# The general attention path's code moved ahead of the banded one's, and the first expert tiles of a two-layer mixture of experts listed half a slot sooner

## The reference

```python
def _attn_ref(q, k, v, n_global, n_local):
    scores = scale * q @ k.T                      # per batch and head
    keep = (pos_k < n_global) | ((rel >= 0) & (rel < n_local))
    scores = np.where(keep, scores - slope[h] * dist, -1e9)
    a = exp(scores - max); a = a / (sum(a) + 1e-09)
    return a @ v

def _moe_ref(x, w_gate, w1, w2):                  # x: 3072 rows of 512
    logits = x @ w_gate                           # 8 experts
    expert_idx = argmax(logits); gate_w = softmax(logits)[expert_idx]
    for e in range(8):
        xe = x[expert_idx == e]
        out[expert_idx == e] = gate_w * (relu(xe @ w1[e]) @ w2[e])
```

## Time and profile before

| | us |
|---|---|
| median of 3 executions | 1014.54 |
| the profiled execution | 1014.87 |
| its span, first to last instruction | 1013.2 |
| outside the span | 1.7 |
| attention, until PE's last attention matmul ends | 279.2 |
| handover, from there to the first down product | 11.0 |
| the rest: two mixtures and what lies between | 723 |

### The profile page before, as it was taken

The page is one execution under the profiler, slowest core; times in us unless marked ns, Lnnn a source line. Parts: engine busy times, 40 slices in busy tenths (PEclk is TensorE's granted clock), DMA queues, the critical chain, the costliest instruction groups (busy, mean ns, idle before and its releaser), DMA issues.

```text
span 1013.2 us, 18862 instructions
## 1 busy us (share of the span) xinstructions
PE 956.1 (94%) x5383; PEld 810.9 (80%) x5384; DVE 609.3 (60%) x1625; ACT 387.9 (38%) x715; POOL 194.7 (19%) x263
## 2 busy tenths in 40 slices
PE   5999999999989999999999999369999999999994
PEld 4999999999868888888888888257888888888883
DVE  5666666667688979879897978872322234222241
ACT  4555555654424433525333333232322233222230
POOL 2002830000122312122221210021221112111110
PEclk9999999999899999999999999779999999999998
DMA  9977974740223515333452515013311115111110
GB/s 166 180 154 186 279 150 98 151 144 17 64 101 140 199 50 207 124 124 126 145 185 77 182 40 199 21 31 115 125 41 45 48 44 197 41 41 41 41 42 9
DMA packets 138412, 110.73 MB, mean 109 GB/s; under 512 B 101839, under 2 KB 114175, under 8 KB 138240
## 3 DMA queue, kind: packets, MB, share of 16 engines
q1 hardware_dynamic: 125808, 74.46, 27.5%
q0 software_dynamic: 11072, 35.69, 10.4%
q10 hardware_dynamic: 1488, 0.04, 0.1%
HBM read 87.36 MB, written 23.33 MB: 109 GB/s over the span
## 4 chain that ended last, share of the span: by engine, by line
PE 90%; DVE 4%; issue 2%; DMA 2%; ACT 1%; DVEq 0%; SPq 0%; POOL 0%; POOLq 0%; ACTq 0%
PE PS L1469 29%; PE PS L1449 29%; PE PS L364 8%; PE PS L342 7%; PE PS L1457 4%; PE PS L352 4%; PE PS L1438 2%; PE PS L299 2%; PE PS L328 2%; PE PS L319 1%; DMA k_rows<-in_k_dram 1%; DMA xin<-attended,early_rows 1%; PE PS L1237 0%; PE PS L1482 0%; DMA xin<-mixed,gather_rows 0%
## 5 line engine op out<-in xcount | busy, mean ns | idle before, releaser
L1449 PE MATMUL PS<-W,xT_high 128*128 (+1 forms) x864 | 272.5, 396 | 3.6 <-DVE xT_low L1617 2.8
L1469 PE MATMUL PS<-W,hT_high 128*128 (+1 forms) x848 | 270.9, 400 | 0.8 <-DVE hT_low L1624 0.8
L1449 PEld LDWEIGHTS PS<-W,xT_high 128*128 128x128 f32 x864 | 159.0, 189 | 35.1 <-issue 3.9
L1469 PEld LDWEIGHTS PS<-W,hT_high 128*128 128x128 f32 x848 | 155.2, 188 | 34.8 <-DVE hT_low L1624 1.0
L1449 PE MATMUL PS<-W,xT_low 128*128 (+1 forms) x432 | 169.3, 392 | 0.0
L1469 PE MATMUL PS<-W,hT_low 128*128 (+1 forms) x424 | 167.6, 395 | 0.0
L1571 ACT ACTIVATE hT_high<-PS 128x512 fp32r<-128x512 f32 x110 | 59.8, 596 | 273.5 <-PE PS L1457 246.5
L1644 DVE CUSTOM_DVE_ANT_0 products<-y,gate_columns 128x512 f32<-128x512 f32 x224 | 141.0, 685 | 0.1
L589 ACT ACTIVATE pbuf<-biased_scores,nmax 128x256 f32<-128x256 f32 (+1 forms) x192 | 87.3, 488 | 105.5 <-DVE nmax L447 104.4
L1566 ACT ACTIVATE h<-PS 128x512 f32<-128x512 f32 x110 | 65.5, 597 | 161.3 <-PE PS L1449 157.6
L1617 DVE TENSOR_TENSOR xT_low<-PS,xT_high 128x512 fp32r<-128x512 f32 x56 | 38.6, 689 | 139.3 <-ACT xT_high L1560 139.0
(11 more groups left out here) (283 smaller groups left out, 1119.5 us busy)
## 6 DMA issues: line engine op xcount, KB each, us to landing
stage<-in_moe_w_dram SPq DMA_DIRECT2D x80, 512.0 KB, 5.5
mixed<-y POOLq DMA_DIRECT2D x30, 256.0 KB, 2.3
q_rows<-in_q_dram SPq DMA_DIRECT2D x32, 192.0 KB, 3.9
k_rows<-in_k_dram SPq DMA_DIRECT2D x32, 192.0 KB, 4.3
v_rows<-in_v_dram SPq DMA_DIRECT2D x32, 192.0 KB
attended<-x_rows SPq DMA_DIRECT2D x16, 384.0 KB, 3.3
v_before<-in_v_dram SPq DMA_DIRECT2D x32, 150.0 KB
stage<-in_moe_w_dram POOLq DMA_DIRECT2D x8, 512.0 KB, 9.3
```

What stands on the lines that cost most here:

```text
L1449: last = pe.matmul(t.PS[:, f, :], lhs[:, c, :], t.W[:, bass.ds(w + part, 512)], start=c == 0 and n == 0, stop=c == KD - 1 and n == 2)
L1469: last = pe.matmul(t.PS[:, 2, :], lhs[:, c, :], t.W[:, bass.ds(off + (c * D + part), D)], start=c == 0 and n == 0, stop=c == KF - 1 and n ...
```

## The change

- The general path's code stands ahead of the banded one on SP, PE, DVE and ACT. Each engine reads the flag once (`path`), ahead of both. What PE and ACT did ahead of the flag (the first transposes and their moves, the waits on constants) is now inside the banded branch; DVE's mask tables (L176 to L182 of the kernel before) become `distances`, called inside the branch. `last_logits` is the end of the banded DVE function.
- `preview_rows` and `preview` part 7 go from slot (3,7) to the end of slot (3,6).
- `turn_first(0)` goes from behind the weighing of head 6 in slot (8,0) to ahead of it, and `x_low_first` on DVE from behind the move of the probabilities to ahead of `finish`. ACT does `x_high_first` ahead of all four parts of `spread_gate2` rather than behind the first.
- The 8 steps of `up_first` stand as 0, 1 / 2 in slot (8,0) and 3, 4 / 5 in slot (8,1), and 6, 7 behind it; before it was none / 0, 1 and 2, 3 / 4, and 5, 6, 7.

```diff
+def path(eng, t, s):
+    eng.wait_ge(s.flag_ready, 1)
+    return eng.to_reg(eng.value_load(t.banded[0:1, 0:1], min_val=0, max_val=1))
...
-    def tensor(pe):
+    def tensor(pe, flag):
...
-        pe.wait_ge(s.ident_made, 2)
-        transpose_qk(0, 0, True, range(4))
-        pe.wait_ge(s.consts, CONSTS)
-        pe.wait_ge(s.qT_cleared, 2)
-        pe.wait_ge(s.small_loaded, 48)
-        pe.wait_ge(s.flag_ready, 1)
-        flag = pe.value_load(t.banded[0:1, 0:1], min_val=0, max_val=1)
-        with pe.If_eq(pe.to_reg(flag), 1):
+        with pe.If_eq(flag, 1):
+            pe.wait_ge(s.ident_made, 2)
+            transpose_qk(0, 0, True, range(4))
+            pe.wait_ge(s.consts, CONSTS)
+            pe.wait_ge(s.qT_cleared, 2)
+            pe.wait_ge(s.small_loaded, 48)
...
+                if not has_h and has_g:
+                    pe.wait_ge(s.xT_moved, 2 * NPR * B - 1)
+                    turn_first(t, s, pe, 0)
                 if has_f:
                     pe.wait_ge(s.pT_moved, 3 * H * b + 2 + 3 * f + 3)
-                    if last and h == 7:
-                        preview_rows(t, s, pe)
                     weigh_v(f % H, range(2, NQ)).then_inc(s.weighed, 1)
                 if not has_h and has_g:
-                    pe.wait_ge(s.xT_moved, 2 * NPR * B)
-                    turn_first(t, s, pe, 0)
                     rank_count(t, s, pe)
                 if not has_h and not has_g:
-                    up_first(t, s, pe, range(2, 4))
+                    up_first(t, s, pe, range(3, 5))
...
                     transpose_p(b, g, 1)
+                    if not has_h:
+                        up_first(t, s, pe, range(0, 2))
...
+                if last and h == 6:
+                    pe.wait_ge(s.logits_moved, NPR * b + 3)
+                    preview_rows(t, s, pe)
                 if has_g:
                     transpose_p(b, g, 2)
...
                 if not has_h:
-                    up_first(t, s, pe, range(0, 2) if has_g else range(4, 5))
+                    up_first(t, s, pe, range(2, 3) if has_g else range(5, 6))
...
-            up_first(t, s, pe, range(5, 2 * KD))
+            up_first(t, s, pe, range(6, 2 * KD))
...
-    def vector(dve):
-        flag = dve.value_load(t.banded[0:1, 0:1], min_val=0, max_val=1)
-        with dve.If_eq(dve.to_reg(flag), 1):
+    def vector(dve, flag):
+        with dve.If_eq(flag, 1):
+            distances(dve)
             dve.sem_inc(s.biased, 3)
...
-                if last and h == 7:
-                    dve.wait_ge(s.weighed, H * b + f + 1)
-                    preview(t, s, dve, 7)
+                if not has_h and has_g:
+                    x_low_first(t, s, dve)
                 if has_f:
                     finish(b, f)
...
                 if not has_h and has_g:
-                    x_low_first(t, s, dve)
                     rank(t, s, dve, 1)
...
+                if last and h == 6:
+                    preview(t, s, dve, 7)
...
             modality(t, s, dve)
+            now = t.logits[:, (B - 1) * NQ:B * NQ, :]
+            dve.wait_ge(s.logits_read, NPR * B)
...
                 if not has_h and has_g:
-                    spread_gate2(act, t, s, range(0, 1))
                     x_high_first(t, s, act)
-                    spread_gate2(act, t, s, range(1, 4))
+                    spread_gate2(act, t, s, range(0, 4))
...
         @block.vector
         def _(dve):
             first_dve(dve)
-            banded_dve(dve)
-            general_dve(dve)
-            last_logits(dve)
+            flag = path(dve, t, s)
+            general_dve(dve, flag)
+            banded_dve(dve, flag)
```

More of the change, by code:

```diff
@@ L98, in sync @@
         sp.sem_inc(s.rows_loaded, 1)
-        sp.wait_ge(s.flag_ready, 1)
     def gpsimd(pool):
@@ L175, in vector, with distances, link @@
         dve.wait_ge(s.tables, TABLES)
+        dve.wait_ge(s.consts, CONSTS)
+    def distances(dve):
+        n = [6]
+        ng, nl = t.parf[:, 0:1], t.parf[:, 1:2]
+        def link(ins):
+            n[0] += 1
+            ins.then_inc(s.setup_chain, 1)
+            dve.wait_ge(s.setup_chain, n[0])
         dist, lost = t.tmp[:, 0, :], t.tmp[:, 2, :]
@@ L247, in gpsimd, with sync @@
         pool.wait_ge(s.x2_cleared, 16 * (MAXT - NT))
-    def sync(sp):
-        flag = sp.value_load(t.banded[0:1, 0:1], min_val=0, max_val=1)
-        with sp.If_eq(sp.to_reg(flag), 1):
+    def sync(sp, flag):
+        with sp.If_eq(flag, 1):
             def load(b, p):
@@ L548, in vector, with scalar @@
             modality(t, s, dve)
-    def scalar(act):
+            now = t.logits[:, (B - 1) * NQ:B * NQ, :]
+            dve.wait_ge(s.logits_read, NPR * B)
+            dve.wait_ge(s.logits_moved, NPR * B)
+            dve.tensor_tensor(now, now, t.ps_lg[:, 0:NQ * E].rearrange("p (i e) -> p i e", e=E), ALU.add)\
+               .then_inc(s.logits_moved, 1)
+            dve.wait_ge(s.logits_moved, NPR * B + 1)
+    def scalar(act, flag):
         def move_qk(b, p, units):
@@ L566, in move_qk @@
                 last.then_inc(s.qk_moved, 1)
-        act.sem_inc(s.qk_moved, 2)
-        move_qk(0, 0, range(4))
-        act.wait_ge(s.consts, CONSTS)
-        act.wait_ge(s.flag_ready, 1)
-        flag = act.value_load(t.banded[0:1, 0:1], min_val=0, max_val=1)
-        with act.If_eq(act.to_reg(flag), 1):
+        with act.If_eq(flag, 1):
+            act.sem_inc(s.qk_moved, 2)
+            move_qk(0, 0, range(4))
+            act.wait_ge(s.consts, CONSTS)
             act.sem_inc(s.exped, 3)
@@ L600, in scalar, with sync @@
             run_slots(act, slot)
[L602 to L612 removed]
+    return gpsimd, sync, tensor, vector, scalar
 def general_attention(t, s, q, k, v, x1, w_gate2):
     qf, kf, vf = (a.rearrange("b h (i p) d -> (b h) p i d", p=P) for a in (q, k, v))
[L619 to L621 removed]
+    def sync(sp, flag):
+        with sp.If_eq(flag, 0):
             sp.sem_inc(s.rows_loaded, 1)
[L624 removed]
             with sp.Fori(0, B) as b:
@@ L642, in sync, with tensor @@
                 sp.dma_start(t.x[:, 0, :], x1[bass.ds(i * P, P), :]).then_inc(s.g_x, 16)
-    def tensor(pe):
-        flag = pe.value_load(t.banded[0:1, 0:1], min_val=0, max_val=1)
-        with pe.If_eq(pe.to_reg(flag), 0):
-            pe.wait_ge(s.qk_moved, 6)
+    def tensor(pe, flag):
+        with pe.If_eq(flag, 0):
+            pe.wait_ge(s.ident_made, 2)
+            pe.wait_ge(s.consts, CONSTS)
+            pe.wait_ge(s.qT_cleared, 2)
+            pe.wait_ge(s.small_loaded, 48)
             with pe.Fori(0, B * H) as n:
@@ L692, in tensor, with scalar @@
             turn_first(t, s, pe, 1)
-    def scalar(act):
-        flag = act.value_load(t.banded[0:1, 0:1], min_val=0, max_val=1)
-        with act.If_eq(act.to_reg(flag), 0):
+    def scalar(act, flag):
+        with act.If_eq(flag, 0):
+            act.wait_ge(s.consts, CONSTS)
             act.sem_inc(s.g_moved, 1)
@@ L713, in scalar, with vector @@
             spread_gate2(act, t, s, range(0, 4))
-    def vector(dve):
-        flag = dve.value_load(t.banded[0:1, 0:1], min_val=0, max_val=1)
-        with dve.If_eq(dve.to_reg(flag), 0):
+    def vector(dve, flag):
+        with dve.If_eq(flag, 0):
             dve.wait_ge(s.rows_loaded, 1)
@@ L1775, in _ @@
             first_loads(sp)
-            banded_loads(sp)
-            general_loads(sp)
+            flag = path(sp, t, s)
+            general_loads(sp, flag)
+            banded_loads(sp, flag)
             sp.wait_ge(s.listed, LISTS)
@@ L1784, in _ @@
         def _(pe):
-            banded_pe(pe)
-            general_pe(pe)
+            flag = path(pe, t, s)
+            general_pe(pe, flag)
+            banded_pe(pe, flag)
             mix_pe0(pe)
@@ L1801, in _ @@
             first_act(act)
-            banded_act(act)
-            general_act(act)
+            flag = path(act, t, s)
+            general_act(act, flag)
+            banded_act(act, flag)
             mix_act0(act)
```

26 lines of the change are left out of this document (5 added, 21 removed).

## The result

The changed kernel takes 1022.13 us (median of 4 runs, 1021.05 to 1023.90) against 1014.72 us of the kernel before beside it (4 runs, 1014.31 to 1015.32): ratio 1.0074, 95% interval 1.0057 to 1.0092. It is 7.4 us slower. The forecast was 1007.9 us, with 0.05 for slower. The profiled execution took 1021.05 us, its span 1019.4 against 1013.2, so the traces hold 6.2 us of the difference.

A forecast was written before the change was run, and what follows sets the result against it. PE was taken to bound the kernel, with DVE some 2 us late at the handover. Gaps -1.5, clock -3.4 and DVE's lateness -1.7 gave -6.6 us, so 1007.9 us, range 1006.6 to 1012.4.

The forecast's parts named there:

- The code order: Start and handover: branches over general code leave the handover; at the start PE's, under 1.4 us, and DVE's cost nothing.
- Rival 2: Start: PE's jump isn't short, PE begins at 11.5 us; +2.4 us on the forecast, 1010.3 us; chance 0.10.
- Rival 4: Start: PE's code fetch waits behind input loads, jump 6.46 + 3.77 = 10.2 us; 1016.7 us; chance 0.05.
- DVE's jump at the start: Start: DVE's branch over the general code takes 2.9 us, hidden because PE's first score waits for ACT until 13.57.
- the terms of the sum: Attention's end and handover: gaps -1.5, clock -3.4, DVE's lateness -1.7, together -6.6 us.
- gaps and clock: PE's end of attention: waits of 2.2 us go, 0.65 is added (-1.5); the clock staying up gives -3.4 us.
- DVE's lateness: Handover: from PE's end to the split second tile, 2.99 us become 1.3, a gain of 1.7 us.
- The early gather: Before slot (8,0): gather issued at 251.9, not 255.00, landing between 255.3 and 258.1, with no PE wait for it.
- rival 1: Attention's end: the clock falls all the same, a little earlier or later; -3.2 us, 1011.3 us; chance 0.27.
- the change of layers: The second low-clock stretch comes here and stays; the clock's rise may shift the time by 1 us either way.
- DVE's jump: Handover: DVE's 3.6 us piece with branch and third flag reading goes from behind attention; not all of it gained.
- 3.4 us of the clock: Attention's end: with PE's gaps gone the clock stays up, -3.4 us; the largest and least sure term.

The follow-up runs named there:

- b1_petail: a3_pad8 with the tail of PE's general path moved behind the banded code under its own test: 1010.79 us, ratio to the kernel before 0.9961.
- b2_pebanded: a3_pad8 with PE's banded code first and its general code behind it: 1010.53 us, ratio to the kernel before 0.9958.
- a4_pad108: The changed kernel with 108 never-executed instructions added to DVE's general path: 1015.18 us, ratio to the kernel before 1.0001.
- a3_pad8: The changed kernel with 8 never-executed instructions added to DVE's general path: 1014.99 us, ratio to the kernel before 1.0000.
- b3_before80: The kernel before with 80 waits on a long-up semaphore spread over DVE's first eight slots: 1023.21 us, ratio to the kernel before 1.0079.
- a1_reorder: The kernel before with only the new order of the last three slots, all code left in place: 1014.22 us, ratio to the kernel before 0.9989.
- c1_oldslots: b2_pebanded with the slot order of the kernel before: 1012.33 us, ratio to the kernel before 0.9979.
- a2_codeorder: The changed kernel with the order of the slots taken back, leaving only the code move: 1025.10 us, ratio to the kernel before 1.0098.

## Why the prediction was wrong

**The failed step** stands in "The code order": the jumps, moved to the start, were to cost nothing. PE's was "I take it to be short", under 1.4 us hidden; it took 4.34 us and cost 3.5. The argument, a few hundred instructions from the first one, was about distance; b1_petail shows that it is about whether the target's block is held: 350 is, 460 is not. Rival 2 (the text on the code order calls it the first) had this mechanism, at the 3.77 us of the earlier trace rows and +2.4 us, with a chance of 0.10. Rival 4's place was right too, its queue of 6.46 us behind the inputs was not: the branch was 0.6 us longer than at the handover.

DVE's jump at the start was mis-sized too, 3.6 to 3.9 us in these kernels for 2.9; in the change PE hid it, in b1_petail and b2_pebanded PE waits 1.3 and 1.0 us for it.

**The larger loss was in no step.** The text followed the code to the start and the handover, and asked nowhere what else on the engines moves with it. Of the 11.6 us 8.4 come from DVE's loop of 300 instructions, which by its new place at 577 lies in four blocks of 128 and not three. What shows it: the stalls at instructions 1 and 5 of the loop, the second at position 581 as that of a4_pad108 is at 709, 128 further; they are gone with 8 dead instructions (a3_pad8), back in part with 108 (a4_pad108), and made in the kernel before with 80 (b3_before80). In the traces DVE's stalls stand beside code packets at 137.2, 141.0 and 143.8 us, and the kernel before has none between 123 and 147. The Trainium skill ("Runtime: NRT & Kernel Launch", Instruction fetch mechanics), on the very page that the prediction used for the jump, gives most engines an instruction memory of 32 KiB, 512 instructions, that is filled as a FIFO. Four blocks of 128 and the one fetched ahead are 640. The runs agree with that size; its blocks of 256 are those of PE here (16 KB packets), while the queue that carries DVE's has packets of 8 KB, half a block. That the loop stalls in four blocks and not in three is shown; that the memory's size is the reason is inferred. A loop of 300 instructions lies in four blocks only if it begins within 44 of a block's end, so no run here parts the count of blocks from a start near such an end.

**What was right.** Taken together, the terms of the sum came nearly as forecast in the change's own trace. From the loop to the end of PE's attention work 11.6 - 7.2 = 4.4 us were won, for 4.9 of gaps and clock; DVE's lateness became 1.42 us for a forecast 1.3, a gain of 1.6 for 1.7. The early gather was issued at 263.5, which is 251.9 and the 11.6 of delay, PE waited for ACT's half of x alone (0.60 us, forecast 0.65), and the clock stayed up (rival 1 falls for the change; in a1_reorder the fall comes 10.8 us later). In a kernel without the two losses, b2_pebanded, PE is 6.05 us ahead of before at the counts, 6.2 at the first down product, 5.5 at 667 us and 4.95 from 700 on, and the span is 4.7 us shorter. At the change of layers the low clock held 30.7 us and not 27.3, and 1.2 us are lost there; the prediction had allowed 1 us either way.

**DVE's jump.** The forecast gave 4.9 us to the order (gaps and clock) and 1.7 to the code. By the ratios, before, a1_reorder, c1_oldslots and b2_pebanded give 1.1 us for the order alone, 2.1 for the code's move without PE's, and 4.3 for both; the intervals (0.2 to 2.0, 1.2 to 3.0, 2.8 to 5.8 us) don't part the 1.1 us of excess from nothing. The traces say more. How late PE is against the kernel before, on the same matmuls:

| Kernel | at 245 us | at the first down product | won |
|---|---|---|---|
| a1_reorder, the order | +0.25 | -1.80 | 2.05 |
| a2_codeorder, the code | +14.07 | +10.22 | 3.85 |
| the change, both | +11.68 | +5.65 | 6.03 |
| c1_oldslots, the code but PE's | -0.13 | -3.27 | 3.14 |
| b2_pebanded, both but PE's code | -0.36 | -6.20 | 5.84 |

So the forecast's 6.6 us came to 6.0, but divided otherwise: the order gave 2.0 and not 4.9, the code 3.9 and not 1.7. The order does put PE's second turn 4.5 us sooner in a1_reorder, and 2.4 us of that go again to the wait for DVE's jump and the half clock there. Neither change alone keeps the clock up: it falls for 6.83 us in a1_reorder, for 3.41 in a2_codeorder and c1_oldslots, and not at all in the drain of the change and b2_pebanded. The step that failed here is to give the whole 3.4 us of the clock to the order. That the total came near is in part luck. The expectations for a1_reorder (4 us) and c1_oldslots (3 to 4) overshot for the same reason, c1_oldslots in its ratio alone.

**What stays open.** Where the code that PE holds at the start ends, between 350 and 460, was not measured more closely. Only one execution of a4_pad108 has a trace, and it is of the slower five of twelve; whether the others have the same stalls is not known. Why the clock's fall in the drain is half as long without DVE's jump was not shown.

## What to carry to other kernels

When code is moved, count where each loop and each branch target lands on every engine, not only where instructions were added: DVE's loop branched back without a stall at 585 and with two at 577, eight instructions earlier. The price was paid at the one branch back that was taken; with more turns it may be paid at each, which no run here shows. A stall on an engine that is 60% busy costs its own length only once the busy engine's queue is empty, and then the clock may double it. And where two waits stand in a row, test them as a square: removing either alone showed 1 to 2 of 4 us, and only the square told which term of the forecast had been given the other's gain.

## What the runs showed that was not expected

- A missing block of code cost DVE 2.9 to 4.0 us (3.12 and 3.33 in the change, 3.31 and 3.62 in a2_codeorder, 3.23 and 2.94 in b3_before80, 4.0 in a4_pad108) and PE 3.4 to 4.4 us, though the packet itself is on the queue for 0.3 to 1.4 us.
- DVE's record of a taken branch is short (67 ns at the start of the change, 69 ns in the loop) and the stall stands behind it as "issue"; PE's record contains it (4341 ns). Looking at branch records alone misses DVE's.
- With a wait of PE of 3.5, 4.1 or 4.4 us in the loop the clock went to its lower level for 10.24 us (b3_before80, the change, a2_codeorder), behind two waits of 1.3 us together for 3.41 us (a4_pad108). In the change the half clock cost as much as the wait itself.
- Behind a jump to near the end of a block, the next block did not come in time: DVE ran into it after 4 instructions (the change) or 11 (b3_before80) and stood still for as long again, after 24 (a4_pad108) for 1.1 us.
